# Loading queries through ScalarE's DMA queue in a fused attention and feed-forward kernel

## What is computed

```python
# attention over pooled keys and values; q, k, v: (4, 8, 576, 64)
k_p = k.reshape(B, H, 72, 8, D).mean(axis=3)
v_p = v.reshape(B, H, 72, 8, D).mean(axis=3)
scores = scale * np.matmul(q, k_p.transpose(0, 1, 3, 2))
attn = softmax(scores)
x = np.matmul(attn, v_p)            # then reshaped to 2304 tokens x 512
# gated feed-forward with RMS norm, d_ff 1536
xn = x / rms * rms_g
x = silu(xn @ w_gate) * (xn @ w_val) @ w_out
# second feed-forward, d_ff 2048
x = silu(x @ w_in) @ w2_out
```

## Time and profile before

| | |
|---|---|
| median of three runs | 881.7 us |
| the profiled execution | 881.81 us |
| its span (first to last instruction on the core) | 879.8 us |
| TensorE busy | 867.8 us, 99% of the span |
| TensorE's granted clock | 1.00 of full speed throughout |
| VectorE, ScalarE, GpSimd busy | 59%, 39%, 39% |
| DMA | 210.55 MB, mean 239 GB/s |

### The profile page before, as it was taken

One profiled execution on the slowest core, in us unless ns is written; L12 is line 12 of the kernel. 1 busy time (PEld: TensorE's weight loads), 2 busy tenths in 40 slices (PEclk: granted clock), 3 DMA queues, 4 the chain that ended last, 5 costly groups with the idle time before them and its releaser, 6 DMA issues.

```text
span 879.8 us, 12937 instructions
## 1 busy us (share of the span) xinstructions
PE 867.8 (99%) x4896; PEld 824.5 (94%) x4896; DVE 520.3 (59%) x834; ACT 347.1 (39%) x653; POOL 343.4 (39%) x360
## 2 busy tenths in 40 slices
PE   7999999999999999999999999999999999999998
PEld 6999999999999999999898999999998989989897
DVE  6689757766557665755654254779655444434432
ACT  3689744542222224345553223135423332322222
POOL 6897999882357673567773000130000000000000
PEclk9999999999999999999999999999999999999999
DMA  9971678778899993656779376766755555474321
GB/s 266 260 204 37 247 274 323 274 282 322 299 346 339 365 344 125 249 198 247 287 301 368 121 256 254 302 257 257 279 207 209 179 201 182 164 267 180 132 96 72
DMA packets 63085, 210.55 MB, mean 239 GB/s; under 512 B 22192, under 2 KB 32432, under 8 KB 49840
## 3 DMA queue, kind: packets, MB, share of 16 engines
q1 hardware_dynamic: 63024, 209.73, 66.1%
HBM read 142.61 MB, written 67.11 MB: 238 GB/s over the span
## 4 chain that ended last, share of the span: by engine, by line
PE 95%; DMA 1%; DVE 1%; SPq 1%; issue 0%; ACT 0%; DVEq 0%; ACTq 0%
PE ps L1654 17%; PE ps L1656 16%; PE ps L1655 16%; PE ps L1723 7%; PE ps L1724 7%; PE ps L1722 7%; PE ps L1698 3%; PE ps L1696 3%; PE ps L1697 3%; PE ps L1583 3%; PE ps L1554 2%; PE ps L1752 2%; PE ps L1753 2%; PE ps L1751 2%; DMA qs<-in_q 1%; PE ps L1566 1%
## 5 line engine op out<-in xcount | busy, mean ns | idle before, releaser
L1654 PE MATMUL ps<-xh,wr 128*128 128x384 f32 x840 | 282.8, 337 | 0.7 <-DVE xacc L1347 0.5
L1656 PE MATMUL ps<-xh,wr 128*128 128x384 f32 x840 | 281.4, 335 | 0.0
L1655 PE MATMUL ps<-xl,wr 128*128 128x384 f32 x840 | 281.1, 335 | 0.0
L1654 PEld LDWEIGHTS ps<-xh,wr 128*128 128x128 f32 x840 | 157.7, 188 | 4.9 <-DVE qt L1297 1.3
L1655 PEld LDWEIGHTS ps<-xl,wr 128*128 128x128 f32 x840 | 157.7, 188 | 0.9
L1656 PEld LDWEIGHTS ps<-xh,wr 128*128 128x128 f32 x840 | 157.7, 188 | 0.0
L1724 PE MATMUL ps<-wo,al 128*128 128x512 f32 x288 | 112.5, 391 | 0.0
L1723 PE MATMUL ps<-wo,ah 128*128 128x512 f32 x288 | 112.4, 390 | 0.0
L1722 PE MATMUL ps<-wo,ah 128*128 128x512 f32 x288 | 112.0, 389 | 0.0
L999 ACT ACTIVATE ah<-qt 128x384 fp32r<-128x384 f32 x96 | 45.3, 518 | 131.1 <-PE ps L1724 126.2
L1334 DVE TENSOR_TENSOR al<-qt,ah 128x384 fp32r<-128x384 f32 x96 | 52.5, 587 | 70.7 <-ACT ah L999 70.5
(11 more groups left out here) (175 smaller groups left out, 1381.8 us busy)
## 6 DMA issues: line engine op xcount, KB each, us to landing
wr<-ring_home SPq DMA_DIRECT2D x40, 1792.0 KB, 7.5
ring_home<-wr SPq DMA_DIRECT2D x20, 1792.0 KB, 8.1
wo<-out_home SPq DMA_DIRECT2D x22, 1024.0 KB, 4.8
out_home<-wo SPq DMA_DIRECT2D x14, 1024.0 KB, 9.1
fw<-fold_home SPq DMA_DIRECT2D x7, 1536.0 KB, 6.3
raw_c<-in_moe_w_out SPq DMA_DIRECT2D x13, 512.0 KB, 8.0
fold_home<-fb SPq DMA_DIRECT2D x6, 1024.0 KB, 8.2
fold_home<-fa SPq DMA_DIRECT2D x6, 768.0 KB, 10.9
```

The costliest lines, as they stand in the source:

```text
L1654: pe.matmul(out_ps, w_hi, x_hi, start=first and c == 0, stop=False, skip_group_check=True)
L1655: pe.matmul(out_ps, w_hi, x_lo, start=False, stop=False, skip_group_check=True)
L1656: ins = pe.matmul(out_ps, w_lo, x_hi, start=False, stop=c == 1, skip_group_check=True)
```

## The change

SP no longer issues the second part of batch 0's keys, nor the queries of tiles 0 to 4; ScalarE's own queue issues them. ScalarE issues keys (1, 3), q0 and q1 at the start of its stream, and q2, q3, q4 behind its copy-out of tiles 0, 1 and 2. SP issues keys and values of batches 0 and 1 and `gT` one after the other, with no wait among them, and takes the queries from tile 5 on.

```diff
+    FIRST_Q = 5
@@ SyncE
                 for i, (lo, hi) in enumerate((KPARTS[:2], VPARTS[:1])[kind] if b == 0 else []):
+                    c0 = hi
+                    if (kind, i) == (0, 1):
+                        continue
                     sp.dma_start(dst[:, lo:hi, :], ...)
-                    c0 = hi
-                if (b, kind) == (0, 1):
-                    load_q(1)
@@
             load_kv(0, 0)
-            load_q(0)
             load_kv(0, 1)
-            load_q(2)
             load_kv(1, 0)
             sp.dma_start(gT[:, :], ...)
-            load_q(3)
             load_kv(1, 1)
             for n in range(4, NT):
-                load_q(n)
+                if n >= FIRST_Q:
+                    load_q(n)
@@ ScalarE
+            def load_q(n):
+                if n >= 2:
+                    act.wait_ge(s_qTm, n - 1)
+                for b, r0, m in parts(n):
+                    s0 = n * P + r0 - b * S
+                    act.dma_start(qs[r0:r0 + m, n % 2, :, :],
+                                  q[b, :, s0:s0 + m, :].rearrange("h s d -> s h d")).then_inc(s_q[n % 2], 16)
+
+            lo, hi = KPARTS[1]
+            act.dma_start(KV[0][0][:, lo:hi, :], k_rows[0, lo * P:hi * P, :].rearrange("(c p) x -> p c x", p=P))\
+               .then_inc(s_kpart[1], 16)
+            load_q(0)
+            load_q(1)
@@
                     act.activation(qT[:, :, :], q_ps, ACT.Copy).then_inc(s_qTc, 1)
+                    if n + 2 < FIRST_Q:
+                        load_q(n + 2)
                     if n in first_tile:
                         keys(first_tile.index(n))
```

More of the change, by code:

```diff
@@ L456, in load_q @@
             def load_q(n):
-                if n >= 2:
-                    sp.wait_ge(s_qTm, n - 1)
+                sp.wait_ge(s_qTm, n - 1)
                 for b, r0, m in parts(n):
```

## The result

The changed kernel takes 885.06 us (median of 15 runs, 883.5 to 886.96), the kernel before 881.7 (15 runs). The ratio is 1.0038, 95% interval [1.0031, 1.0044]: slower by 3.4 us. The forecast was 880.7, a gain of 1.0; the time lies within the stated range, but on the other side of the kernel before and almost at the value of rival A (885.1). The profiled execution took 884.43 us, with a span of 882.4.

A forecast was written before the change was run, and what follows sets the result against it. TensorE, busy 99% of the span, was taken as the bound, so only its waits before 26 us counted. The terms -0.94 - 0.28 + 0 + 0.19 gave -1.03 us, hence 880.7 us, range 879.5 to 885.8.

The forecast's parts named there:

- rival A: Early loads: engines alternate between both queues packet by packet, so q0 and q1 land late; +3.4 us, 885.1; chance 0.30.
- likeliest case: Whole kernel: the forecast itself, 880.7 us, own range 879.5 to 881.8; chance 0.42.
- edit 5: SP's stream: early loads follow without a wait, batch 1's keys come earlier; no time of its own.
- edit 1: Tile 4's queries: q4 on ScalarE's queue removes TensorE's 0.96 us wait; -0.94 us.
- Edit 2: Values of batch 0: they come earlier, so VectorE begins their sum without its 0.28 us idle; -0.28 us.
- Edit 3: Front, batch 0's keys and q0: earlier issue against shared DMA engines; taken as 0, ends -0.45 and +1.6 us.
- Edit 4: DMA issues on ScalarE: q2's issue delays the copy of `kT`; +0.19 us.
- Rival B: ScalarE's issue of q2 takes 2.3 us, delaying the copy of `kT`; sum +1.0 us, 882.7; chance 0.13.

The follow-up runs named there:

- e12: The changed kernel once more, unaltered, as a second profiled execution; 886.82 us.
- e2: The changed kernel, but SP holds only the values of batch 1 until ScalarE has copied out tile 0's queries; 885.02 us, ratio 1.0035.
- e5: The changed kernel with 31 more identity transposes on TensorE where it stood idle; 885.21 us, ratio 1.0037.
- e7: The kernel before with q2 alone on ScalarE's queue, SP issuing the keys of batch 1 at the same moment; 885.52 us, ratio 1.0041.
- e9: As e7, but SP holds the keys of batch 1 so that they are issued after q2; 882.01 us, ratio 1.0003 against the kernel before.
- e1: The changed kernel, but SP holds keys and values of batch 1 until ScalarE has copied out tile 0's queries; 884.07 us, ratio 1.0023.
- e4: The kernel before with only q4's two DMAs on ScalarE's queue, behind its copy of tile 2; 881.21 us, ratio 0.9994.
- e3: The kernel before with only the second part of batch 0's keys on ScalarE's queue; 881.52 us, ratio 0.9994.
- e6: The kernel before with 23 more warm-up transposes on TensorE, loads unchanged; 884.25 us, ratio 1.0027.

## Why the prediction was wrong

**The likeliest case failed in edit 5**, "SP's own stream: all its early loads follow without a wait", which the prediction counted as "cover for edit 1, no time of its own". I had taken the free run of SP for a cover, and the sum never asked when q1 and q2 would land beside it. SP's waits for the buffers of q2 and q3 had held the 2.4 MB of batch 1 back in the kernel before, and so had kept the way free for q1, q2 and q3. The term that is missing is the late landing of these queries:

- q2 landed at 18.4 us instead of 14.3. At tile 0's product that is 1.46 us beyond what VectorE's blocks would have cost (2.16 - 0.70), but only some 0.4 beyond ScalarE's copy of `prT`, which the lower clock had made late.
- q1 landed at 9.8 in the first profiled execution, and at 14.1 to 14.7 in e12, e2 and e5, where TensorE waited 1.4 to 2.1 us for it. It was 10.8 in the kernel before.
- TensorE, left idle for much of 6.6 to 10.9 us, was then granted half the clock for some 7 us (0.53 from 11 to 18 us), which the sum had at nothing too.

That the order of issue makes q2 late, and that this alone can cost 3.5 us, e7 and e9 show. That it is not the whole difference in the changed kernel e1 shows, where q2 was in time and 1.3 of 3.4 us came back.

**Edit 1** was right in that the wait goes, wrong in size: -0.36 us (e4), because the copy of prT is what is late next, a wait that I didn't look up in TensorE's stream. The list of waits was also read too short: between the rows shown in the earlier trace rows stand 1.3 us for VectorE's `pr` ahead of tile 1's scores and 1.1 us for `xacc` at 352 us. **Edit 2** held: VectorE's sum of the values starts at 14.22 with no wait ahead of it; what that saves is not shown, as the scores before it were late themselves. **Edit 3** was inside its bounds but not at 0: +0.56 us in the changed kernel (+0.77 in e12), while with the keys alone (e3) chunk 4 landed at 6.98 us, as in the unchanged kernel (7.36 and 6.93). q0 and q1, moved ahead of chunk 4, are the likely reason. **Edit 4** cost nothing: ScalarE issued q2 at 9.03, before its copy of `qT` even started (9.24), and `kT` was copied by both engines at the same moment. Rival B did not occur; no issue on ScalarE took over 0.7 us.

**Rival A** had nearly the time, and in part the mechanism. It let q0 land at 13.1; it landed at about 7.6, ahead of the last keys: in the first 8 us ScalarE's small packets did not take turns with SP's, they went ahead (1028 against 66). It foresaw a late q1 (19.0); that was 14.1 to 14.7 in three of four executions and 9.8 in the other. And it had no term for q2. Its range for the sum (+2.9 to +3.9) and the measured +3.4 agree in part by luck: the two profiled executions have +1.7 and +3.9 at 26 us, and each lost about 1 us more later. The Trainium skill's rule ("DMA: Bandwidth & Descriptors", section "Queues, rings and completion order": an engine goes round the queues packet by packet) is borne out from 13 us on, with one row of 64 or 512 elements to a packet, 210 against 235. It does not describe 5.0 to 6.2 us, nor 9.5 to 13.0, where a queue with a DMA issued moved nothing, nor e9, where 1040 packets of q2 moved beside 72. In each of these most of the packets were those of the load that had been issued first, if only by half a microsecond. The order of issue does not explain everything either: from 6 to 8 us ScalarE's queue moved 1023 packets, q1's for the most part, and SP's 103, though the last keys had been issued 0.1 us ahead of q1. The counts show all this, the mechanism they don't.

What stays open: how the 3.4 us divide between q1, q2, the keys and the clock over many executions, since q1's landing changes from one to the next; and e6.

## What to carry to other kernels

A wait that one queue makes on behalf of a small load is also what keeps the large loads behind it away: before moving the small load to another queue, ask for every load on the path what will be issued ahead of it and beside it, and when it lands. If it is moved, hold the large loads back until it is issued (e9: one wait, 3.5 us), and do so for every small load behind it too: in e1 q2 was saved and q3 was late instead. And when a wait goes, look up all semaphores that the instruction behind it waits for, not only those that show in the profile.

## What was not expected of the hardware

- Two DMAs on two queues, issued at 9.10 (1 MB in rows of 2 KB) and 9.11 us (256 KB in rows of 256 bytes): the small one landed 9.8 us after its issue. Issued 0.6 us ahead of the large one, 5.2 us.
- A DMA on ScalarE's queue issued at 9.03 us had its first packet moved at about 13.1, while SP's, issued before it, moved 623 from 9.5 to 13.0.
- From then on about as many packets of each queue moved, 210 of 256 bytes beside 235 of mostly 2 KB. Earlier (5.0 to 6.2 us) it was 1028 against 66, in e9 1040 against 72: taking turns is not what the two queues always do.
- q1, issued at 1.82 or 1.83 us in two executions of the same kernel, landed 7.9 us after its issue in one and 12.6 in the other.
- Issuing a DMA on ScalarE took 0.37 to 0.7 us, and began before the activation ahead of it in the stream had started (9.03 against 9.24), so it cost that engine nothing.
- After a standstill of 3.60 us TensorE's granted clock was 0.50 from 19 to 22 us (e7), and the product of 12 matmuls took 2.80 us, in the kernel before 1.74.
